# Gate and value products of pairs of token blocks by seven half-size products with mixed weights kept in DRAM

## What is computed

```python
gate = 1.0 / (1.0 + np.exp(-(x @ w_gate)))   # 512 x 1536
val = x @ w_val                               # 512 x 1536
return gate * val @ w_out                     # 1536 x 512
```

## Time and profile before

| | us |
|---|---|
| median of three runs (lowest, highest) | 1631.28 (1630.37, 1633.56) |
| own time of the profiled execution | 1633.38 |
| its span, first to last instruction | 1631.4 |
| TensorE busy | 1505.4, 92% of the span |
| VectorE, ScalarE, POOL busy | 584.1, 380.4, 311.8 |
| DMA, mean over the span | 76 GB/s |

### The profile page before, as it was taken

How to read it: one execution, slowest core, us unless ns; L and a number is a source line. 1 busy time by engine, 2 the same in 40 slices (tenths; PEclk the granted TensorE clock), 3 DMA queues, 4 the chain that set the end, 5 groups by cost and what they waited for, 6 DMA issues and landing times.

```text
span 1631.4 us, 25528 instructions
## 1 busy us (share of the span) xinstructions
PE 1505.4 (92%) x8836; PEld 1234.1 (76%) x8837; DVE 584.1 (36%) x1095; ACT 380.4 (23%) x698; POOL 311.8 (19%) x402
## 2 busy tenths in 40 slices
PE   5765549999999999989999999999999999999997
PEld 4544438888888888868888888888888888888885
DVE  4444366457645665334411212122121211212111
ACT  4443312222221212223311211112121111212111
POOL 0223354444444444310000000000000000000000
PEclk8676559999999999999999999999999999999998
DMA  9555234245423443315300201002010100100000
GB/s 330 202 210 187 72 124 146 75 116 150 127 84 97 138 122 96 102 57 127 80 27 1 52 1 27 27 2 51 0 27 27 27 26 0 27 26 1 26 0 26
DMA packets 78612, 124.07 MB, mean 76 GB/s; under 512 B 17342, under 2 KB 41918, under 8 KB 78528
## 3 DMA queue, kind: packets, MB, share of 16 engines
q1 hardware_dynamic: 56576, 80.85, 16.8%
q0 software_dynamic: 17216, 39.75, 7.6%
q10 hardware_dynamic: 4736, 2.26, 0.6%
HBM read 91.38 MB, written 32.52 MB: 76 GB/s over the span
## 4 chain that ended last, share of the span: by engine, by line
PE 88%; issue 6%; DVE 2%; ACT 1%; DMA 1%; another core or an unknown queue 1%; SPq 0%; POOLq 0%; POOL 0%; ACTq 0%; DVEq 0%
PE ps L1136 37%; PE ps L1147 18%; PE ps L1112 13%; PE ps L1090 13%; PE ps L1042 2%; PE ps L1099 2%; PE ps L1029 1%; PE ps L1006 1%; DMA vt<-in_v 1%; ACT qp L584 0%; DVE ew L746 0%; DMA x_rows<-zero 0%; DVE xb L815 0%; DVE ssum L828 0%
## 5 line engine op out<-in xcount | busy, mean ns | idle before, releaser
L1136 PE MATMUL ps<-yhi,gv 128*128 128x512 f32 x1728 | 557.0, 393 | 6.5 <-DVE wo L967 5.8
L1136 PEld LDWEIGHTS ps<-yhi,gv 128*128 128x128 f32 x1728 | 325.3, 188 | 79.2 <-DVE wo L967 6.2
L1136 PE MATMUL ps<-ylo,gv 128*128 128x512 f32 x864 | 339.4, 393 | 0.0
L1147 PE MATMUL ps<-wo,shi 128*128 128x512 f32 x864 | 266.8, 390 | 1.4 <-DVE slo L984 1.4
L982 DVE TENSOR_TENSOR s<-ps,sig 128x512 f32<-128x512 f32 x108 | 74.7, 691 | 472.0 <-ACT sig L666 467.3
L1090 PE MATMUL ps<-ew,xhi 128*128 x640 | 202.4, 397 | 4.5 <-DVE xlo L891 3.2
L529 POOL DMA_INDIRECT out<-ot,out_tok x36 | 34.5, 960 | 870.4 <-ACT ot L681 864.6
L1112 PE MATMUL ps<-ew,hhi 128*128 x640 | 197.1, 389 | 1.3 <-DVE hlo L908 1.3
L1136 PEld LDWEIGHTS ps<-ylo,gv 128*128 128x128 f32 x864 | 162.6, 188 | 37.8 <-issue 1.1
L1147 PEld LDWEIGHTS ps<-wo,shi 128*128 128x128 f32 x864 | 162.1, 188 | 36.9 <-DVE slo L984 1.9
L666 ACT ACTIVATE sig<-ps 128x512 f32<-128x512 f32 x108 | 64.5, 597 | 494.8 <-PE ps L1136 486.1
(11 more groups left out here) (159 smaller groups left out, 1214.8 us busy)
## 6 DMA issues: line engine op xcount, KB each, us to landing
raw<-in_moe_w SPq DMA_DIRECT2D x64, 512.0 KB
xg<-x_rows POOLq DMA_DIRECT2D x160, 64.0 KB
kt<-in_k SPq DMA_DIRECT2D x8, 1152.0 KB, 5.7
vt<-in_v SPq DMA_DIRECT2D x8, 1152.0 KB, 9.6
qt<-in_q SPq DMA_DIRECT2D x8, 1152.0 KB, 5.4
yin<-y_rows SPq DMA_DIRECT2D x32, 256.0 KB, 5.3
graw<-in_moe_w_gate SPq DMA_DIRECT2D x6, 512.0 KB, 3.8
graw<-in_moe_w_val SPq DMA_DIRECT2D x6, 512.0 KB, 4.8
```

Source lines behind the costliest of these rows:

```text
L1136: last = mm(ps[:, 2 * (f % 2) + part, :], gv[f // 2][:, w, part, d, cols], x[c % 2][:, d, :], start=first, stop=end)
L1147: last = mm(ps[:, 4 + m, :], s[:, rows], wo[f // 2][:, w, f % 2], start=(f == 0 and s is shi and w == 0), stop=(f == GC - 1 and s is slo))
```

## The change

Block 0 stays as it was. Blocks 1 to 8 go in four pairs ("supers"). With the tokens of the two blocks as one half index, the two halves of the width as the other, and gate and value as columns, the 2x2 by 2x2 product of a slice is made by the Winograd form of Strassen's scheme: seven products of half the width and fifteen additions. Four of the seven weights are differences of gate and value quarters (t1 and t3 made by POOL, t2 and t4 by VectorE), split once, in block 0, into high and low parts; they and the plain ones are stored to DRAM (`mixes`, 3584 columns a slice) and loaded again for each step into one of two buffers st. The seven token operands (a_in, then a_hi and a_lo) are made once for a pair. A step of a pair is seven products in four PSUM banks by turns, one copy from PSUM (z, ScalarE) and seven additions (VectorE), two sigmoids and two multiplications. The first block's result s0 goes on to `output` at once; the second block's, s1, is kept for all twelve slices, and its twelve outputs follow. shi and slo have two buffers; `keep_out` waits for each output bank alone.

```diff
+    MIX = 2 * 768 + 4 * 512
+    SUPERS = (NB - 1) // 2
...
+    RAW_AT = [1, 6, 7, 5, 2, 4, 8]
+    RAW_FIRST = [8, 8, 9, 9, 9, 9, 10, 10]
+    RAW_A = [0, 0, 1, 2, 3, 3, 4, 5]
+    HIGH_A = [2, 4, 5, 6, 7, 8, 9]
+    PRODUCTS = [256, 2560, 2048, 1536, 512, 3072, 0]
...
+    gv = [Place(ew_base + 16384 * n)(f"gv{n}", [128, 2, 2, 2, DC, 128], F32R) for n in range(4)]
+    high_part = Place(ew_base + UNITS * 2 * 4096)
+    at4 = high_part.at
+    gv += [high_part(f"gv{n}", [128, 2, 2, 2, DC, 128], F32R) for n in (4, 5)]
+    wo = [high_part(f"wo{n}", [128, 2, 2, D], F32R) for n in range(PIECES)]
+    at_mix = high_part.at
+    mix = high_part("mix", [128, 2, 4, 2, 2, 128], F32R)
...
+    a_hi = first_part("a_hi", [128, 7, 2, BLK], F32R)
+    a_in = Place(first_part.at)("a_in", [128, 7, 2, BLK], F32)
+    a_lo = first_part("a_lo", [128, 7, 2, BLK], F32R)
...
+    st = [Place(at4 + 16384 * n)(f"st{n}", [128, MIX], F32R) for n in range(2)]
...
+        def bank_of(f, idx):
+            return ps[:, (7 * f + idx) % 4, :]
+        def outs_before(i, step):
+            return GC + 2 * GC * i + step
...
             def load_glu(n):
+                if n > 0:
+                    sp.wait_ge(glo_made, 3 * n - 1)
+                    sp.wait_ge(t13_made, 2 * n)
+                    sp.wait_ge(t24_made, 2 * n)
+                cols = slice(256 * n, 256 * n + 256)
+                sp.dma_start(graw[:, 0], gate_v[:, :, cols]).then_inc(graw_in, 16)
+                sp.dma_start(graw[:, 1], val_v[:, :, cols]).then_inc(graw_in, 16)
+            def load_wo(n):
                 wait(sp, glo_made, 3 * n)
-                cols = slice(256 * n, 256 * n + 256)
-                sp.dma_start(graw[:, 0, :].rearrange("p (c f) -> p c f", c=DC), gate_v[:, :, cols]).then_inc(graw_in, 16)
-                sp.dma_start(graw[:, 1, :].rearrange("p (c f) -> p c f", c=DC), val_v[:, :, cols]).then_inc(graw_in, 16)
-                sp.dma_start(graw[:, 2, :].rearrange("p (c f) -> p c f", c=2), wo_v[:, 2 * n:2 * n + 2, :]).then_inc(graw_in, 16)
-
-            def load_y(b):
-                sp.wait_ge(yt_made, 4 * b)
+                sp.dma_start(wraw[:], wo_v[:, 2 * n:2 * n + 2, :]).then_inc(wraw_in, 16)
+            def store_plain(n):
+                sp.wait_ge(glo_made, 3 * n + 2)
+                for w in range(2):
+                    src = gv[n][:].bitcast(F32).rearrange("p f w s d x -> p f w (s d x)")[:, :, w, 256:1024]
+                    dst = mixes[2 * n:2 * n + 2, :, 768 * w:768 * w + 768].rearrange("f p x -> p f x")
+                    sp.dma_start(dst, src).then_inc(b_out if n < 4 else b_out_late, 16)
+            def store_mixes(n):
+                for op in range(4):
+                    sp.wait_ge(tlo_made, 4 * n + op + 1)
+                    at = 1536 + 512 * op
+                    sp.dma_start(mixes[2 * n:2 * n + 2, :, at:at + 512].rearrange("f p x -> p f x"),
+                                 mix[:, :, op].bitcast(F32).rearrange("p f w k x -> p f (w k x)")).then_inc(t_out[op], 16)
+            def load_y(i, t):
                 for g in range(4):
-                    sp.dma_start(yin[32 * g:32 * g + 32], y_v[b, g]).then_inc(yin_in, 16)
+                    sp.dma_start(yin[t][32 * g:32 * g + 32], y_v[1 + 2 * i + t, g]).then_inc(yin_in0 if t == 0 else yin_in1, 16)
             tiles_used = sp.value_load(used[0:1, 0:1], min_val=FULL, max_val=NT)
-            tiles_early = sp.value_load(used[0:1, 1:2], min_val=E - 1, max_val=NT)
-            sp.wait_ge(pe_y, tiles_early)
             load_glu(0)
-            load_glu(1)
             sp.wait_ge(pe_y, tiles_used)
             for p in range(2):
                 sp.wait_ge(y_out[p], (tiles_used + (1 - p)) // 2 * 16)
-            load_glu(2)
+            load_wo(0)
             sp.dma_start(out_tok[:], out_tok_v, allow_slow_non_contiguous=True).then_inc(tok_in, 16)
-            load_y(1)
-            for n in range(3, PIECES):
-                load_glu(n)
-            for b in range(2, NB):
-                load_y(b)
+            for n in range(PIECES):
+                store_plain(n)
+                if n + 1 < PIECES:
+                    load_glu(n + 1)
+                if n == 0:
+                    sp.wait_ge(yt_made, 4)
+                    load_y(0, 0)
+                if n + 1 < PIECES:
+                    load_wo(n + 1)
+                else:
+                    sp.wait_ge(t13_made, 2 * PIECES)
+                    sp.wait_ge(t24_made, 2 * PIECES)
+                    load_y(0, 1)
+                store_mixes(n)
+            sp.wait_ge(b_out, 16 * 8)
+            sp.wait_ge(b_out_late, 16 * 4)
+            for op in range(4):
+                sp.wait_ge(t_out[op], 16 * PIECES)
+            for n in range(SUPERS * GC):
+                if n < 2:
+                    sp.wait_ge(pe_gv, 10 + 2 * n)
+                else:
+                    sp.wait_ge(pe_p, 7 * (n - 1))
+                sp.dma_start(st[n % 2][:].bitcast(F32), mixes[n % GC]).then_inc(st_in[n % 2], 16)
+                if n % GC == 3 and n // GC + 1 < SUPERS:
+                    sp.wait_ge(a_raw, 8 * (n // GC) + 4)
+                    for t in range(2):
+                        load_y(n // GC + 1, t)
             for m in range(4):
                 sp.wait_ge(o_out[m], 16 * NB)
...
+            for n in range(PIECES):
+                pool.wait_ge(graw_in, 32 * (n + 1))
+                for op, (a, b) in enumerate(((quarter(1, 0), quarter(0, 0)), (quarter(1, 1), quarter(1, 0)))):
+                    wait(pool, t_out[op], 16 * n)
+                    nc.gpsimd.tensor_tensor(mix[:, :, op, 1].bitcast(F32), a, b, ALU.subtract).then_inc(t13_made, 1)
...
             def keep_out(b):
-                act.wait_ge(pe_o, GC * (b + 1))
                 for m in range(4):
+                    if m < 3:
+                        act.wait_ge(pe_bank, 3 * b + m + 1)
+                    else:
+                        act.wait_ge(pe_o, GC * (b + 1))
                     wait(act, o_out[m], 16 * b)
                     nc.scalar.copy(ot[:, m], ps[:, 4 + m, :]).then_inc(o_kept, 1)
...
+                for f in range(GC):
+                    wait(act, s_made, f)
+                    act.wait_ge(pe_gv, f + 1)
+                    nc.scalar.activation(sig[:], ps[:, 2 * (f % 2), :], ACT.Sigmoid).then_inc(sig_made, 1)
+                    wait(act, pe_o, f)
+                    act.wait_ge(s_made, f + 1)
+                    nc.scalar.copy(shi[0][:], s32[:]).then_inc(shi_made, 1)
+                    if f % 3 == 0 and f < 9:
+                        if f > 0:
+                            high_out(f // 3 * 2)
+                        high_mix(f // 3 * 2)
+                    if f % 3 == 1 and f < 9:
+                        high(f // 3 * 2 + 1)
+                        high_out(f // 3 * 2 + 1)
+                    if f % 3 == 2 and f < 9:
+                        high_mix(f // 3 * 2 + 1)
+                        if f < 8:
+                            high(f // 3 * 2 + 2)
+                        else:
+                            high_a(0, 0)
+                    if f >= 10:
+                        for idx in range(1 + 3 * (f - 10), 4 + 3 * (f - 10)):
+                            high_a(0, idx)
+            def super_step(i):
+                more = not isinstance(i, int) or i + 1 < SUPERS
+                for f in range(GC):
+                    n, k = GC * i + f, outs_before(i, f)
+                    wait(act, s0_made, n)
+                    act.wait_ge(pe_p, 7 * n + 1)
+                    nc.scalar.copy(z[:], bank_of(f, 0)).then_inc(z_made, 1)
+                    act.wait_ge(c11_made, n + 1)
+                    nc.scalar.activation(z[:], z[:], ACT.Sigmoid).then_inc(sig0_made, 1)
+                    act.wait_ge(c21_made, n + 1)
+                    nc.scalar.activation(u3[:], u3[:], ACT.Sigmoid).then_inc(sig1_made, 1)
+                    act.wait_ge(pe_o, k if f == 0 else k - 1)
+                    act.wait_ge(s0_made, n + 1)
+                    nc.scalar.copy(shi[f % 2][:], u2[:, f % 2]).then_inc(shi_made, 1)
+                    if f == 0:
+                        keep_out(2 * i)
+                for j in range(GC):
+                    k = outs_before(i, GC + j)
+                    act.wait_ge(pe_o, k - 1)
+                    act.wait_ge(s1_made, GC * i + j + 1)
+                    nc.scalar.copy(shi[j % 2][:], s1_of(j)).then_inc(shi_made, 1)
+                    if j == 0:
+                        keep_out(2 * i + 1)
+                    if more and j in HIGH_A:
+                        high_a(i + 1, HIGH_A.index(j))
+                if not more:
+                    keep_out(2 * i + 2)
...
+            def mixes_of(n):
+                wait(dve, t_out[2], 16 * n)
+                dve.wait_ge(t13_made, 2 * n + 1)
+                nc.vector.tensor_tensor(mixed(2), quarter(1, 1), mixed(0), ALU.subtract).then_inc(t24_made, 1)
+                wait(dve, t_out[3], 16 * n)
+                dve.wait_ge(t24_made, 2 * n + 1)
```

(127 more changed lines are left out.)

249 lines of the change are left out of this document (139 added, 110 removed).

## The result

The median is 1574.2 us (1571.4 to 1575.6, four runs) for 1632.3 us of the kernel before beside it: a ratio of 0.9643, 95% interval 0.9625 to 0.9660, 58 us faster. The profiled execution has a span of 1569.7 us and an own time of 1571.4.

A forecast was written before the change was run, and what follows sets the result against it. TensorE, busy 92% of the span, was taken as the bound. Fewer matmuls 74.4 plus the end 2.1, less block 0 15.0 and clock 2, gave 59.5 us off 1631.3: 1572 us, range 1557 to 1600.

The forecast's parts named there:

- Fewer matmuls: Blocks 1 to 8: 42 product matmuls for 48 per step, 288 fewer, at 0.2267 us each; gain 74.4 us.
- Rival (a): Pairs: products run at block 2's slow cadence, 0.2329 us; 12.5 us less gain, 1585 us; chance 0.17.
- The four hand-overs: Last f of each pair's first half: only output(10) covers VectorE's work; 0.4 us wait each, 1.6 us in all.
- VectorE's combination hidden: Pair steps: VectorE's ten operations stay under 8 of 12.2 us, so no product waits for them.
- Rival (e): Pairs: VectorE bounds the step, needing over 1.1 us per operation; 1620 us; chance 0.05.
- The stream of weights hidden: Pairs: each 1.84 MB st loads in 5.3 us of 15 available; up to 2 us per pair if yin is slower.
- Block 0, 17.3 us longer and 2 for the clock forecast: Block 0: queue traffic delays its end, 116.6 us for 99.3; 2 us more for half-speed clock after waits.
- The pace of 15.3 us a piece: Block 0: queue repeats every 15.3 us per piece at 342 GB/s; TensorE waits at f=2, 4, 6, 9.
- rival (b): Block 0: landing, mixes_of, load and casts uncovered, queue empty 3.5 us in each piece; +21 us, 1593; chance 0.20.
- Rival (c): Block 0: stores to DRAM slower than loads, at 162 GB/s; +71.6 us, 1643; chance 0.05.
- (d): Block 0: queue moves 387 GB/s, saving 10.3 us, and no clock is lost; 1560 us; chance 0.17.
- The end: Final output: copies go bank by bank, so the last send starts 2.1 us earlier; gain 2.1 us.

The follow-up runs named there:

- the eighth product: Changed kernel with product 3 made twice in each step; first product to last matmul 791.3 us, 64.3 more; kernel 1640 us, one run.
- the two runs: Changed kernel with four and eight more VectorE operations of 128x512 per step; first product to last matmul 729.7 and 766.6 us, 2.8 and 39.7 more.
- the second run: Changed kernel run again unchanged; block 0 113.9 us, first product to last matmul 727.0 us; 0.961 of the kernel before.
- the reordered one: Changed kernel, block 0 mixes of pieces 1, 3, 5 one slice later, split of pieces 2, 4 before the next sigmoid; block 0 114.6 us, ratio 0.963.
- the first run: Changed kernel as first measured against the kernel before; median 1574.2 us, ratio 0.9643; block 0 113.1 us, first product to last matmul 726.9 us.

## Why the prediction was right

It forecast 1572 us and the kernel takes 1574.2; the sum was 59.5 us, and the profiled execution is 61.7 us shorter. The mechanism of each term held, but part of the closeness is luck: the pairs gained 4.4 us less than forecast, block 0 lost 5.5 us less, and 1.2 us come from the stage before, whose last matmul ended at 717.70 for 718.95 us; no run tells whether that is the other order of loads ahead of block 0 or chance.

**Fewer matmuls, 74.4 forecast, 70.0 measured.** The count and the cadence of the products were right (0.2267 us, the eighth product's 65.4 us for 65.3). Rival (a), the slow cadence, is out. The term is 4.4 us too large by terms beside it. 2.4 us are slo0 at the top of a partition, since the prediction looked at a_hi and a_lo alone; the run with slo0 moved shows them. One wait of product 5 of the first pair, whose sum u2 stands behind five low parts of the first pair on VectorE (the prediction took those to be in time without following u2 behind them), costs 1.1 us from start to start. The four hand-overs cost 0.5 us each from start to start, 2.0 for the 1.6 forecast. That makes 3.9; the other 0.5 us, under 0.1% of the stretch, are not traced.

**VectorE's combination hidden**: shown, with the slack bounded from both sides by the two runs. Rival (e) is out.

**The stream of weights hidden**: shown. The changed kernel has no wait for st in the pairs, and two yin between two st (11 us of issue at 1038.7) did no harm. For st 0 it is close: in the second run it landed at 784.2, 1.1 us before the first product, and in the reordered one it was 1.3 us late.

**Block 0, 17.3 us longer and 2 for the clock forecast, 13.8 with the clock measured.** The pace of 15.3 us a piece was right to 0.5 us, the places of TensorE's waits too: they are in slices 2, 6, 7 and 9 in the first run and in the forecast's 2, 4, 6 and 9 in the second. But that pace is luck in part: it came from one rate of 342 GB/s for everything, and the 341 measured over two pieces are stores at 405 to 419 and slower loads taken together. The size was off for two reasons. The queue was done 6 us sooner (last mix store landed at 825.7 for 832): the last piece's loads were asked 2.3 us sooner, of which 1.1 is the earlier start, and the last piece and its yin took 4 us less than forecast. And the last slices, which stand behind no store, cover the end, so st 0 wasn't what the first product waited for. The account behind the number was too simple as well: the queue's bytes and the chain through the one mix buffer are nearly as long as each other, which rival (b) had named, so that fewer bytes gain little. Had the chain been followed alone, from one ask to the next, it would have come to 14.4 to 15.1 us a piece (699.62, 714.75 and 729.13 without the plain stores). Rival (c), slow stores, is out, and (d), 387 GB/s, came true for the stores but not for whole pieces. For the clock 2 us were forecast; TensorE's wait from 737.0 to 740.8 was followed by 5.3 us at 1.2 GHz (to 746.1), which costs half of it, 2.7, and the three others kept 2.4 GHz.

The Trainium skill ("TensorE: Matmul & The Clock Gate", HAM oscillation) would have the clock go only after long waits. The changed kernel's first profile agrees; its second one and others don't (last section).

**The end, 2.1 us**: 2.0 measured.

What stays open: why matmuls are 0.003 to 0.012 us slower when an operand lies at the top of a partition, from where on, and why the outputs took 2.76 us when yhi1 lay there, since ot and yin had moved too. And whether two mix buffers would free block 0 was not tried: there is no place for a second one of 16 KB in its SBUF.

## What to carry to other kernels

When a matmul count is what sets the end, price a change of algorithm by count times the distance of matmuls in the trace, and then ask only whether the other engines' work fits beside one step; adding idle work to an engine until the time moves gives the slack from both sides. A single buffer that is refilled only after its store has landed makes a chain as long as the queue itself: count the bytes and the chain both, and the larger one is the price, since taking bytes away helps only down to the chain. Work that is moved within an order written by hand moves the wait with it when something else is the pace.

## What the runs showed of the hardware

**The clock after a wait.** In the changed kernel's second run TensorE waits for 2.0 us from 734.3 on (length, busy of PE, PE clock, share, GB/s):

```profile
734.00:735.00 1.00, 0.27 (x2) 1.00 0.44 172
...
736.00:737.00 1.00, 0.74 (x3) 1.00 1.00 341
737.00:738.00 1.00, 1.00 (x4) 0.62 1.09 383
738.00:739.00 1.00, 1.00 (x3) 0.50 1.15 269
```

and goes on at 1.2 GHz until 740.6; after a wait of the same length at 763.6 it keeps 2.4, as the first profile did after its waits of 2.0 to 2.3 us. In the reordered run one of 1.79 us (to 745.68) lost it; with slo0 alone moved waits of 3.43 us (to 685.95) and 2.75 us (to 705.66) kept it. So in that span of 1.8 to 3.4 us the length of a wait doesn't tell whether the clock falls, and each slow stretch of 3.4 us costs block 0 half of that, 1.7 us, in one run and not in another of the same program; what tells is open. The changed kernel's waits of 3.75 us (first run) and 4.0 (second) lost it.

**Rates of the queue.** Large stores from SBUF to DRAM (2 and 3 KB rows) moved 405 to 419 GB/s at full share, loads of 1 and 2 KB rows 311 to 359. But the loads of st, with rows of 14 KB, moved 444 and 452 GB/s in the two microseconds from 1078 and from 1284 of the changed kernel. So it may be the length of the rows and not the direction that tells stores and loads apart; no run changes one of them alone.

**POOL beside VectorE.** A POOL subtraction of 128x512 with two inputs from SBUF took 1.29 us with no VectorE operation beside it (at 747.61) and up to 2.39 beside VectorE's, and some of VectorE's were stretched as well (ns min/median/max, changed kernel):

```profile
L608 POOL TENSOR_TENSOR mix<-graw x12: 1257/1426/2389, 720.8 to 810.0; 128x512 f32<-128x512 f32 x12
L1118 DVE TENSOR_TENSOR mix<-graw,mix x6: 678/776/1698, 731.3 to 810.5; 128x512 f32<-128x512 f32 x6
```

0.69 us became up to 1.70; in the run where VectorE made all mixes the same six took 0.685 to 0.695. The Trainium skill ("GPSIMD Engine Reference", Elementwise) puts such an operation at an estimated 1.1 us; the trace has 1.29 without a neighbour. The same page's specifications say that the two engines share the SBUF interface with two SBUF inputs, and the trace agrees.
